# A three-stage kernel (attention, experts, dense layer): a later wait on ScalarE, a turned expert loop, and a dense layer whose two matmul kinds alternate in longer runs

## The chip, the cores and the metric

The kernel runs on one core of a Trainium2 chip. The metric is the device time of one execution in microseconds, as the median of several. Five engines run side by side, each with its own instruction list: TensorE (PE, matrix products), VectorE (DVE), ScalarE (ACT), GpSimd (POOL) and SyncE (SP, which here only starts transfers). They meet through semaphores.

## The reference, cut to what matters

```python
x = attention(q, k, v)                       # pooled attention + a band of |i-j| < 4
x = reshape(x)                               # 2304 tokens x 512
expert = argmax(x @ w_gate); gate = softmax at that expert      # 8 experts
x[rows of e] = gate * (relu(xe @ w1[e]) @ w2[e])                # 512 -> 1024 -> 512
h = x @ w_in                                 # dense layer, 512 -> 2048
g = where(h >= 1, h, where(h <= -1, 0, (h + 1)**2 / 4))
out = g @ w_out                              # 2048 -> 512
```

All inputs and outputs are float32.

## The kernel before, in words

The first 215 us or so are the attention and the routing, which the change does not touch.

**Split products.** From the expert stage on, each operand stands as a high part and a low part, both in a 32-bit format that PE multiplies at a single pass, and one product is three matmuls: high by high, low by high, high by low (`three`, lines 1303 to 1305). ACT makes the high part of each 128x512 weight chunk (line 675), POOL the low part (line 466), and `lo_done` counts the chunks that are ready.

**The expert stage.** Tokens are sorted by expert into slots of 128 rows; there are up to 25 slots, of which 21 (numbers 0 to 20) are in use with these inputs. For a slot s PE runs four steps: `turn_x` (four transposes of the rows), `hidden` (24 matmuls with 512 columns, into two banks), `turn_h` (eight transposes of the hidden values) and `project` (24 matmuls, into one bank). They are pipelined over slots: after a lead-in, PE's order is hidden(s), turn_x(s+1), project(s-1), turn_h(s), and then hidden(s+1). The loop is `Fori(1, 24)` with an `If(s < end)` around its body, where `end` (20 here) is read from a table; so at the end four trips run through with nothing in them. The last slot stands behind the loop. `weights_of(s)` reads two table entries (which expert, which half of the weight memory) into registers; it stands before each `hidden` and each `project`. DVE, SP and ACT have loops of the same kind. SP stores each slot's rows (line 401), waits for the landing, and after its own empty trips it raises `all_stored` (line 417).

**The dense layer.** The tokens are in six groups of three tiles of 128 rows. For a group, f counts 16 blocks of 128 hidden columns. `hidden2(f)` is 12 matmuls with 384 columns into one of two banks (output name tp). Then a chain makes the activation: DVE clamps (line 1078), ACT squares (line 767), DVE combines (line 1082, `act_done`), ACT casts the high part (line 769), POOL subtracts the low part (line 571, `act_lo`). `rows(f)` is 9 matmuls with 512 columns into three banks, one for each tile (output names sc and pt). PE's order is hidden2(f), then rows(f-2); `hidden2(f)` waits for `act_done` of f-2, because it writes that bank anew. At the end of a group stand rows(13), rows(14), rows(15), and then hidden2 of blocks 0, 1 and 2 of the next group. At f = 8 to 11 PE also turns a quarter of the next group's rows (`turn_x2`, three transposes, line 1384), and DVE splits it (`split_x2`). In the first group ACT and POOL still prepare chunks 8 to 15 of `w_out` between their other work. At a group's end ACT copies the three tiles out (`take_group`, line 762) and POOL scatters them to their rows by three indirect transfers (line 566).

**The wait on all_stored.** Buffers of the dense layer lie where the slots' rows lay until they are stored. ACT waits for `all_stored` ahead of the first group's whole work; DVE waits for it ahead of act_f of f = 2.

The orders are written out by hand; nothing reorders them.

Of the kernel before, what the change touches and what calls it, by code (L numbers as in the profile page):

```python
# [52 lines left out]
KD = DM // P  # L53
# [26 lines left out]
def write_program(nc, ctx, q, k, v, w_gate, w1, w2, w_in, w_out, out, x_nat, y_rows):  # L80
# [516 lines left out]
    def _(act):  # L597
# [157 lines left out]


        def take_group(g):
            if not (isinstance(g, int) and g == 0):
                act.wait_ge(rows_stored, 16 * GT * g)
            for n in range(GT):  # L760
                act.wait_ge(o_full, GT * g + n + 1)
                act.copy(rows_out[:, n, :], o_ps[n][:]).then_inc(o_evac, 1)
# [9 lines left out]
            take_group(g)  # L772

        act.sem_inc(o_evac, GT)
        act.wait_ge(all_stored, 1)
        group(0, True)
        with act.Fori(1, GROUPS) as g:
            group(g)
# [3 lines left out]
    def _(dve):  # L782
# [280 lines left out]
        def split_x2(g, par, k):  # L1063
            n = KD * g + k + 1
            turned = (x2T_first[k] if isinstance(g, int) and g == 0 else x2T_ps[k % 2])[:, 0:GT * P]
            dve.wait_ge(x2T_full, n)
            dve.tensor_copy(x2T[par][:, 0, k, :], turned).then_inc(x2T_hi, 1)
            dve.wait_ge(x2T_hi, n)
            dve.tensor_tensor(x2T[par][:, 1, k, :], turned, x2T[par][:, 0, k, :], ALU.subtract).then_inc(x2T_done, 1)

        def group(g, par, last):


            for f in range(KFF):
                n = KFF * g + f + 1
                src = h2_ps[f % 2][:, 0:GT * P]
                dve.wait_ge(h2_full, n)
                dve.tensor_scalar(clamped[f % 2][:], src, -1.0, 1.0, ALU.max, ALU.min).then_inc(clamp_done, 1)  # L1078
                dve.wait_ge(square_done, n)
                if isinstance(g, int) and g == 0 and f == 2:  # L1080
                    dve.wait_ge(all_stored, 1)
                dve.scalar_tensor_tensor(act_f[f % 4][:], src, -1.0, clamped[f % 2][:], ALU.max, ALU.add).then_inc(act_done, 1)  # L1082
                if not last:
                    if 8 <= f < 8 + KD:
                        split_x2(g + 1, 1 - par, f - 8)

        dve.wait_ge(y_stored, 16 * 12)
        for k in range(KD):
# [11 lines left out]
    def _(pe):  # L1100
# [206 lines left out]
        def weights_of(s):  # L1307
            c = pe.value_load(slot_cs[0:1, bass.ds(s, 1)], min_val=0, max_val=E - 1)
            par = pe.value_load(slot_par[0:1, bass.ds(s, 1)], min_val=0, max_val=1)
            return c, par  # L1310
# [4 lines left out]
        def turn_x(s):  # L1315
            pe.wait_ge(xs_done, s + 1)
            if not (isinstance(s, int) and s == 0):
                pe.wait_ge(xT_done, s)
            for k in range(KD):
                e = pe.transpose(xT_ps[:, k * P:(k + 1) * P], xs[:, k * P:(k + 1) * P], ident[:])  # L1320
            e.then_inc(xT_full, 1)

        def hidden(s, c, par):
            pe.wait_ge(xT_done, s + 1)
            if not (isinstance(s, int) and s == 0):
                pe.wait_ge(relu_done, 2 * s)
            for k in range(KD):
                for half in range(2):
                    n = 2 * k + half
                    pe.wait_ge(lo_done, NCH * c + n + 1)  # L1330
                    e = three(h_ps[half][:], lambda part: xT[:, part, k * P:(k + 1) * P],
                              lambda part: chunk(par, part, n), k == 0, k == KD - 1)
                    if k == KD - 1:
                        e.then_inc(h_full, 1)
# [25 lines left out]
        turn_h(0)  # L1360
        keep_clock(sc[1], SPARE // 2)

        def slot(s, last):
            hidden(s, *weights_of(s))
            if not last:
                turn_x(s + 1)
            project(s - 1, *weights_of(s - 1))
            turn_h(s)

        end = pe.value_load(last_slot, min_val=TILES - 1, max_val=SLOTS - 1)  # L1370
        with pe.Fori(1, SLOTS - 1) as s:
            with pe.If(s < end):
                slot(s, False)
        slot(end, True)

        def turn_x2(g, par, k):
            first = isinstance(g, int) and g == 0
# [23 lines left out]
                          lambda part: x2T[par][:, part, k, :], k == 0, k == KD - 1)  # L1401
            e.then_inc(h2_full, 1)

        def rows(g, f):
            pe.wait_ge(act_lo, KFF * g + f + 1)
            if isinstance(g, int) and g == 0:
                pe.wait_ge(lo_done, NCH * (E + 1) + f + 1)
            for i in range(GT):
                if f == 0:
                    pe.wait_ge(o_evac, GT * g + i + 1)  # L1410
                e = three(o_ps[i][:], lambda part: act_s[f % 4][:, part, i * P:(i + 1) * P],
                          lambda part: wts[:, 1, part, f * CH:(f + 1) * CH], f == 0, f == KFF - 1)
                if f == KFF - 1:
                    e.then_inc(o_full, 1)

        def group(g, par, last):
            for f in range(KFF + 2):
                if f < KFF:
                    hidden2(g, par, f)
                if f >= 2:  # L1420
                    rows(g, f - 2)
                if not last and 8 <= f < 8 + KD:
                    turn_x2(g + 1, 1 - par, f - 8)

        group(0, 0, False)
        with pe.Fori(0, GROUPS // 2 - 1) as i:
            group(2 * i + 1, 1, False)
            group(2 * i + 2, 0, False)
        group(GROUPS - 1, 1, True)


_INS = ["q", "k", "v", "moe_w_gate", "moe_w1", "moe_w2", "moe2_w_in", "moe2_w_out"]
# [19 lines left out]
```

## Time and profile before

| | |
|---|---|
| median of 3 runs | 918.72 us (917.51 to 921.9) |
| profiled execution, its own time | 921.8 us |
| its span | 919.9 us |
| mean granted PE clock | 0.982 |
| PE busy | 871.2 us, 95% of the span |
| POOL, DVE, ACT busy | 49%, 49%, 40% |

All times in rows are microseconds from the span's start. PE's matmuls overlap, so the distance between starts tells the pace, and not the duration that a row shows. A bracket at the end of a timeline row is the time in which the engine stood idle ahead of it, and what ended it; "issue" means that the profile shows nothing that it waited for. A bracket may be short of the distance between starts, since the rows' durations include the draining of the last matmul. L-numbers are lines of the kernel.

### The profile page before, as it was taken

To read this page: it belongs to the slowest core of one execution; us is meant where nothing else is said; L and a number is where in the kernel's file an instruction comes from. 1 tells how busy PE (TensorE), PEld (TensorE's weight loads), DVE (VectorE), ACT (ScalarE), POOL (GpSimd) and SP (SyncE) were. 2 spreads that over 40 slices of the span, in tenths; PEclk is the share of its full clock that TensorE was granted. 3 is DMA by queue.
4 is the path that set the end of the run, shared out by engine and by line. 5 is a ranking of instruction groups with operands and counts; after the bars stand their busy time and mean duration, and the time that the engine had idled before them with its cause. 6 is when DMAs were issued, how large, how long until landed. Compare 5 with 4: busy or idle time off the path is not lost.

```text
span 919.9 us, 17885 instructions
## 1 busy us (share of the span) xinstructions
PE 871.2 (95%) x5190; PEld 750.4 (82%) x5191; DVE 447.7 (49%) x1192; ACT 369.2 (40%) x1013; POOL 450.2 (49%) x470
## 2 busy tenths in 40 slices
PE   6999999956998999999998999999999999999995
PEld 5878888845785888888877998999989999899995
DVE  3888888866554545554544242242242242242221
ACT  5888888841322443234222423323223223223222
POOL 4556555665987886588444631421422322322322
PEclk9999999986999999999999999999999999999998
DMA  7355666444776665466434200100200100200000
GB/s 159 78 136 139 148 146 167 116 120 115 217 231 170 197 197 163 128 199 205 137 115 119 101 1 1 70 1 0 70 1 1 69 0 0 69 0 0 35 1 35
DMA packets 109992, 88.71 MB, mean 96 GB/s; under 512 B 67904, under 2 KB 81728, under 8 KB 109952
## 3 DMA queue, kind: packets, MB, share of 16 engines
q10 hardware_dynamic: 23040, 41.95, 15.4%
q1 hardware_dynamic: 83472, 34.87, 14.5%
q0 software_dynamic: 3440, 11.38, 3.9%
q8 instruction: 22, 0.36, 0.2%
q14 instruction: 18, 0.15, 0.0%
HBM read 73.07 MB, written 15.10 MB: 96 GB/s over the span
## 4 chain that ended last, share of the span: by engine, by line
PE 85%; POOL 5%; DMA 3%; issue 3%; DVE 2%; ACT 1%; SPq 0%; ACTq 0%; POOLq 0%; DVEq 0%
PE tp L1303 10%; PE tp L1305 10%; PE tp L1304 10%; PE sc L1138 5%; PE pt L1305 5%; PE pt L1304 5%; PE pt L1303 5%; PE xo L1303 4%; PE xo L1305 3%; PE xo L1304 3%; POOL wts L466 3%; PE tp L1215 3%; PE sc L1304 2%; PE sc L1305 2%; PE sc L1303 2%
## 5 line engine op out<-in xcount | busy, mean ns | idle before, releaser
L571 POOL TENSOR_TENSOR act_s<-act_f,act_s 128x384 fp32r<-128x384 f32 x96 | 97.4, 1015 | 285.5 <-ACT act_s L769 285.4
L466 POOL TENSOR_TENSOR wts<-stage,wts 128x512 fp32r<-128x512 f32 x160 | 205.3, 1306 | 64.7 <-ACT wts L675 58.8
L675 ACT CAST wts<-stage 128x512 fp32r<-128x512 f32 x160 | 98.5, 621 | 206.6 <-DMA stage<-in_moe_w 90.9
L1078 DVE TENSOR_SCALAR clamped<-tp 128x384 f32<-128x384 f32 x96 | 53.5, 558 | 195.9 <-PE tp L1305 195.9
L767 ACT ACTIVATE clamped<-clamped,mhalf 128x384 f32<-128x384 f32 x96 | 59.2, 617 | 217.8 <-DVE clamped L1078 208.4
L1303 PE MATMUL tp<-x2T,wts 128*128 128x384 f32 x384 | 132.1, 344 | 2.7 <-DVE act_f L1082 2.7
L1305 PE MATMUL tp<-x2T,wts 128*128 128x384 f32 x384 | 129.8, 338 | 0.0
L1304 PE MATMUL tp<-x2T,wts 128*128 128x384 f32 x384 | 129.5, 337 | 0.0
L1082 DVE SCALAR_TENSOR_TENSOR act_f<-tp,clamped 128x384 f32<-128x384 f32 x96 | 53.5, 558 | 68.9 <-ACT clamped L767 68.9
L1303 PEld LDWEIGHTS tp<-x2T,wts 128*128 128x128 f32 x384 | 72.6, 189 | 6.5 <-DVE act_f L1082 3.0
L1303 PE MATMUL tp<-wts,xT 128*128 x168 | 68.7, 409 | 7.6 <-POOL wts L466 4.9
L1305 PE MATMUL pt<-wts,act_s 128*128 128x512 f32 x192 | 75.8, 395 | 0.0
L1304 PE MATMUL pt<-wts,act_s 128*128 128x512 f32 x192 | 75.5, 393 | 0.0
L1304 PEld LDWEIGHTS tp<-x2T,wts 128*128 128x128 f32 x384 | 72.7, 189 | 2.8
L1303 PE MATMUL pt<-wts,act_s 128*128 128x512 f32 x192 | 74.5, 388 | 0.0
L616 ACT ACTIVATE prob<-prob,nmax 96x112 f32<-96x112 f32 x192 | 71.8, 379 | 4.0 <-DVE nmax L809 2.9
L769 ACT CAST act_s<-act_f 128x384 fp32r<-128x384 f32 x96 | 49.3, 514 | 59.9 <-DVE act_f L1082 59.9
L1305 PEld LDWEIGHTS tp<-x2T,wts 128*128 128x128 f32 x384 | 72.6, 189 | 0.0
L1303 PE MATMUL xo<-wts,hT 128*128 x168 | 67.5, 402 | 2.1 <-issue 1.6
L1304 PE MATMUL tp<-wts,xT 128*128 x168 | 66.2, 394 | 0.0
L1305 PE MATMUL tp<-wts,xT 128*128 x168 | 66.1, 394 | 0.0
L1305 PE MATMUL xo<-wts,hT 128*128 x168 | 65.7, 391 | 0.0
(187 smaller groups left out, 1678.0 us busy)
## 6 DMA issues: line engine op xcount, KB each, us to landing
stage<-in_moe_w ACTq DMA_DIRECT2D x128, 256.0 KB, 3.0
y_rows<-xg SPq DMA_DIRECT2D x21, 260.0 KB, 3.5
vw<-in_v SPq DMA_DIRECT2D x96, 56.0 KB
x<-y_rows SPq DMA_DIRECT2D x6, 780.0 KB, 4.5
qn<-in_q SPq DMA_DIRECT2D x32, 144.0 KB, 3.3
kn<-in_k SPq DMA_DIRECT2D x32, 144.0 KB, 3.2
v<-in_v SPq DMA_DIRECT2D x16, 288.0 KB
x_nat<-xb SPq DMA_DIRECT2D x16, 288.0 KB, 4.0
```

The source lines that it names most:

```text
L466: pool.tensor_tensor(wts[:, par, 1, cols], stage[:, n % STG, :], wts[:, par, 0, cols], ALU.subtract).then_inc(lo_done, 1)
L571: pool.tensor_tensor(act_s[f % 4][:, 1, :], act_f[f % 4][:], act_s[f % 4][:, 0, :], ALU.subtract).then_inc(act_lo, 1)
L616: e = act.activation(prob[par][g][:, i, :], prob[par][g][:, i, :], ACT.Exp, bias=nmax[par][:, 3 * g + i:3 * g + i + 1], scale=-1.0, accum_ ...
L675: act.copy(wts[:, par, 0, n * CH:(n + 1) * CH], stage[:, n % STG, :]).then_inc(hi_done, 1)
L767: act.activation(clamped[f % 2][:], clamped[f % 2][:], ACT.Square, bias=mhalf[:], scale=0.5).then_inc(square_done, 1)
L769: act.copy(act_s[f % 4][:, 0, :], act_f[f % 4][:]).then_inc(act_hi, 1)
L1078: dve.tensor_scalar(clamped[f % 2][:], src, -1.0, 1.0, ALU.max, ALU.min).then_inc(clamp_done, 1)
L1082: dve.scalar_tensor_tensor(act_f[f % 4][:], src, -1.0, clamped[f % 2][:], ALU.max, ALU.add).then_inc(act_done, 1)
L1138: e = pe.matmul(sc[g % 2][0:TQ, i * W:(i + 1) * W], qT[par][D * hh:D * hh + D, TQ * t:TQ * t + TQ], kT[par][D * hh:D * hh + D, WSTART[t]:W ...
L1303: pe.matmul(o, stationary(0), moving(0), start=start, stop=False)
L1304: pe.matmul(o, stationary(1), moving(0), start=False, stop=False)
L1305: return pe.matmul(o, stationary(0), moving(1), start=False, stop=stop)
```

## The change

ACT's wait for `all_stored` goes from ahead of the first group to that group's `take_group`. In the expert stage hidden(1) is drawn ahead of PE's loop, and a trip is now turn_x(s+1), project(s-1), turn_h(s), hidden(s+1); behind the loop stand project(end-1) and turn_h(end). In the dense layer PE's f goes in steps of two: hidden2(f), hidden2(f+1), rows(f-2), rows(f-1); the turns stand at f = 8, 10, 12, 14, and DVE's splits at f = 9, 11, 13, 15. In the last group the last six triples of matmuls are reordered: block 14 for tiles 0 and 1, block 15 for tile 0, block 14 for tile 2, block 15 for tiles 1 and 2.

```diff
@@ ACT
         def take_group(g):
-            if not (isinstance(g, int) and g == 0):
+            if isinstance(g, int) and g == 0:
+                act.wait_ge(all_stored, 1)
+            else:
                 act.wait_ge(rows_stored, 16 * GT * g)
...
         act.sem_inc(o_evac, GT)
-        act.wait_ge(all_stored, 1)
         group(0, True)
@@ DVE
-                    if 8 <= f < 8 + KD:
-                        split_x2(g + 1, 1 - par, f - 8)
+                    if f >= 9 and f % 2 == 1:
+                        split_x2(g + 1, 1 - par, (f - 9) // 2)
@@ PE
-        def slot(s, last):
-            hidden(s, *weights_of(s))
-            if not last:
-                turn_x(s + 1)
-            project(s - 1, *weights_of(s - 1))
-            turn_h(s)
-
         end = pe.value_load(last_slot, min_val=TILES - 1, max_val=SLOTS - 1)
+        hidden(1, *weights_of(1))
         with pe.Fori(1, SLOTS - 1) as s:
             with pe.If(s < end):
-                slot(s, False)
-        slot(end, True)
+                turn_x(s + 1)
+                project(s - 1, *weights_of(s - 1))
+                turn_h(s)
+                hidden(s + 1, *weights_of(s + 1))
+        project(end - 1, *weights_of(end - 1))
+        turn_h(end)
...
-        def rows(g, f):
+        def rows(g, f, tiles=range(GT)):
...
-            for i in range(GT):
+            for i in tiles:
...
         def group(g, par, last):
-            for f in range(KFF + 2):
+            for f in range(0, KFF + 2, 2):
                 if f < KFF:
                     hidden2(g, par, f)
-                if f >= 2:
+                    hidden2(g, par, f + 1)
+                if f >= 2 and not (last and f >= KFF):
                     rows(g, f - 2)
-                if not last and 8 <= f < 8 + KD:
-                    turn_x2(g + 1, 1 - par, f - 8)
+                    rows(g, f - 1)
+                if not last and 8 <= f < 8 + 2 * KD:
+                    turn_x2(g + 1, 1 - par, (f - 8) // 2)
...
         group(GROUPS - 1, 1, True)
+        rows(GROUPS - 1, KFF - 2, (0, 1))
+        rows(GROUPS - 1, KFF - 1, (0,))
+        rows(GROUPS - 1, KFF - 2, (2,))
+        rows(GROUPS - 1, KFF - 1, (1, 2))
```

## Rows read from the trace of the kernel before

**Rows 1.** PE's waits: releaser, total us, times, longest us.
```profile
PE tp L1303 <- POOL wts L466: 4.9, 9, 1.5
```
**Rows 2.** Timeline at the first dense group: start, duration, engine, what, [idle].
```profile
500.36 0.56 DVE L1078 TENSOR_SCALAR clamped<-tp 128x384 f32<-128x384 f32 x1 [1.29 <-PE tp L1305]
...
501.99 0.34 PE L1305 MATMUL tp<-x2T,wts 128*128 128x384 f32 x1
...
503.75 0.61 ACT L767 ACTIVATE clamped<-clamped,mhalf 128x384 f32<-128x384 f32 x1 [9.36 <-SPq L417]
...
504.40 0.56 DVE L1082 SCALAR_TENSOR_TENSOR act_f<-tp,clamped 128x384 f32<-128x384 f32 x1 [3.48 <-ACT clamped L767]
...
505.01 0.62 PE L1303 MATMUL tp<-x2T,wts 128*128 128x384 f32 x1 [2.68 <-DVE act_f L1082]
...
508.76 0.40 PE L1303 MATMUL sc<-wts,act_s 128*128 128x512 f32 x1
```
**Rows 3.** The windows view: busy time by engine, granted clock, DMA share, GB/s.
```profile
477.00:484.00 7.00, 7.00 (x24) 5.57 (x25) 1.18 (x3) 0.00 (x0) 0.00 (x0) 0.76 0.02 7
505.00:508.30 3.30, 3.29 (x10) 3.29 (x11) 0.97 (x2) 2.56 (x5) 2.72 (x3) 0.52 0.93 301
```
**Rows 4.** The chain of waits: the last slot's store.
```profile
499.35 2.10 DMA y_rows<-xg
```
**Rows 5.** PE's timeline at the loop's end, slots 19 and 20.
```profile
474.08 1.03 PE L1343 MATMUL pt<-ident,hs 128*128 128x128 f32 x8
476.96 0.49 PE L1303 MATMUL tp<-wts,xT 128*128 x1 [1.84 <-issue]
...
484.18 0.39 PE L1303 MATMUL xo<-wts,hT 128*128 x1
...
489.62 1.03 PE L1343 MATMUL pt<-ident,hs 128*128 128x128 f32 x8
```
**Rows 6.** The same in the trip whose hidden step had waited for POOL's weights.
```profile
294.17 0.60 PE L1320 MATMUL sc<-ident,xs 128*128 128x128 f32 x4
295.59 0.49 PE L1303 MATMUL xo<-wts,hT 128*128 x1 [0.83 <-issue]
...
301.17 1.03 PE L1343 MATMUL pt<-ident,hs 128*128 128x128 f32 x8
301.95 0.48 PE L1303 MATMUL tp<-wts,xT 128*128 x1
```
**Rows 7.** PE's timeline at the end of the first group: blocks' first matmuls.
```profile
564.42 0.39 PE L1303 MATMUL sc<-wts,act_s 128*128 128x512 f32 x1
...
566.50 0.39 PE L1303 MATMUL sc<-wts,act_s 128*128 128x512 f32 x1
...
570.58 0.33 PE L1303 MATMUL tp<-x2T,wts 128*128 128x384 f32 x1
...
572.69 0.33 PE L1303 MATMUL tp<-x2T,wts 128*128 128x384 f32 x1
...
574.77 0.41 PE L1303 MATMUL tp<-x2T,wts 128*128 128x384 f32 x1
...
576.95 0.39 PE L1303 MATMUL sc<-wts,act_s 128*128 128x512 f32 x1
```
**Rows 8.** PE's timeline around one turn in the second group.
```profile
604.15 0.49 PE L1384 MATMUL sc<-ident,x 128*128 128x128 f32 x3
604.40 0.42 PE L1303 MATMUL tp<-x2T,wts 128*128 128x384 f32 x1
...
606.57 0.39 PE L1303 MATMUL sc<-wts,act_s 128*128 128x512 f32 x1
```
**Rows 9.** Timelines of ACT and POOL at the kernel's end.
```profile
909.17 0.59 ACT L762 COPY rows_out<-sc 128x512 f32<-128x512 f32 x1 [2.46 <-PE sc L1305]
...
910.59 1.01 POOL L566 DMA_INDIRECT out_rows<-rows_out,tok_i  x1 [2.78 <-ACT rows_out L762]
911.90 0.97 POOL L566 DMA_INDIRECT out_rows<-rows_out,tok_i  x1 [0.30 <-issue]
```

## The prediction

> **What bounds the kernel now.** I read the page first: PE is busy for 95% of the span, and in the dense stage its digits stand at 9 throughout while no other engine passes 50%. So the end is set by PE, and only three things can move it: PE's idle time, its clock, and the pace at which its matmuls follow each other. The waits view then tells how little idle time is left. The largest in the two stages that the change touches is nine waits for POOL's weights, 4.9 us together, the longest 1.5 [rows 1]; the reader should see in the other two (2.68 us for DVE's act_f [rows 2], 1.84 us of issue [rows 5]) that each is a single event, so the timeline around each one tells its cause. Behind both, the windows view shows the granted clock down: mean 0.52 over 505 to 508.3, which is the 1.2 GHz level, and 0.76 over 477 to 484, a mix of the two levels [rows 3].
>
> **Part A, ACT's wait.** The clamp of f = 0 ended at 500.36 + 0.56 = 500.92. ACT squared it only at 503.75, when SP raised all_stored [rows 2]; SP's last store had been issued at 499.35 and landed 2.10 later, at 501.45 [rows 4], and 2.3 us went on its empty trips. DVE's act_f came at 504.40, and PE, whose last matmul before had started at 501.99 and which would have gone on 0.17 later at 502.16, began the third block at 505.01 [rows 2]: 2.85 us lost. Its twelve matmuls then took 508.76 - 505.01 = 3.75 us at the low clock [rows 2, 3], where the same third block of the next group took 576.95 - 574.77 = 2.18 [rows 7]. With the wait moved, the square follows the clamp at once: 500.96, act_f at about 501.6 to 502.2, PE at about 502.25. That is the usual start of a group, where the third block follows with next to no stall (572.69 to 574.77 is a full block, and the first matmul of the third shows some 0.1 of wait) [rows 7]. New end of that block: 502.16 + 2.18 = 504.34, against 508.76: **4.4 us**.
> What is late next: DVE still waits for all_stored ahead of act_f of f = 2. That block's clamp can't start before its 12 matmuls end (about 504.5) and act_f follows some 1.3 later, about 505.8; the flag stands at 503.75. Two microseconds of cover, so this wait costs nothing, and an expert stage that ends earlier moves both alike. Queued behind ACT's moved wait is only the copy of the first group's tiles, 60 us later. Cast and chunk work of f = 0 also comes earlier, and the later chunks' loads with it. Bounds: 0, if the other wait took over; 4.4. I take 4.4.
>
> **Part B, the turned loop.** PE's matmuls are the same ones in the same order; what moves is where the loop's edge, its test, and the empty trips stand. At the usual edge (turn_h, edge, two table reads, hidden) PE loses nothing: eight transposes from 301.17, and hidden at 301.95 [rows 6]. So the sequencer runs ahead of the array by at least the edge and two reads. At the loop's end it has four empty trips as well, and there the transposes from 474.08 end their turn at 8 x 0.109 = 0.87 later, 474.95, and hidden starts at 476.96 [rows 5]: 2.0 us lost. How far ahead it is, in instructions, the trace doesn't show, but it cancels: before, the last instructions ahead of the empty trips are eight transposes at 0.11 us; now they are matmuls of hidden at 0.227 (5.44 us for 24, 484.18 to 489.62 [rows 5]). A lead of between 8 and 24 matmuls is worth 8 x (0.227 - 0.109) = 0.95 us more than before. The stall shrinks from 2.0 to about **1.05 us**. The lead itself: SP's four empty trips took 2.3 [rows 2, 4], two reads take 0.8 to 1.4 (idle between turn_x and project behind a wait, 294.17 to 295.59 [rows 6]), so some 3.4 us, less the stall of 2.0: 1.4 us ahead, that is 8 transposes and 2 or 3 matmuls, inside those limits.
> Then the clock. After 2.0 us of nothing behind 0.87 us of transposes, hidden took 484.18 - 476.96 = 7.22 us, at a mean granted clock of 0.76 [rows 3, 5]; a hidden step at full clock takes about 5.55 (24 x 0.231, the pace of these steps). The pause at 294.17 (transposes, then 0.83 us idle and a start 1.0 late) was followed by a project step of 5.58 us, 295.59 to 301.17 [rows 6], which is the full level. A stall of 1.05 with dense matmuls on both sides is nearer to that one: I take the clock as kept, gaining 1.67. Bounds 0 and 1.67.
> Price: in the trip whose hidden step waits for POOL chunk by chunk, the sequencer is not ahead. Now the edge comes right behind it, ahead of turn_x and project's two reads, and adds itself to the 295.59 start: a trip's edge is about the 2.3/4 = 0.6 us that SP took for an empty one [rows 4]; I take 0.45, bounds 0 and 0.6. Everything ahead of that trip is absorbed by POOL, whose low parts wait for gathers and not for PE [rows 1]. Sum of B: 0.95 + 1.67 - 0.45 = **2.2 us**, bounds -0.6 and 3.6.
>
> **Part C, longer runs.** The distances between blocks' first matmuls show a price for changing kind. rows(13), right behind a hidden2, took 566.50 - 564.42 = 2.08; rows(14) and (15), behind rows, 570.58 - 566.50 = 4.08, 2.04 each. hidden2(0) behind rows took 572.69 - 570.58 = 2.11, hidden2(1) behind hidden2 574.77 - 572.69 = 2.08 [rows 7]. The finer distances fit: behind a change, and there alone, some ten matmuls are irregular. So a change costs 0.041 us into rows and 0.025 into hidden2, to within the 10 ns of a row. Before, a group has 14 of each; now 7 of each. Saved: 7 x 0.066 = 0.46 us a group. Against it, the fourth turn now stands between rows(13) and rows(14). A turn is 0.25, and hidden2 behind it 2.17 (604.15, 604.40, 606.57 [rows 8]); rows behind transposes may cost 5.58 - 5.44 = 0.14 [rows 5, 6] over an undisturbed block, so this turn costs about 0.07 more than it did. Five groups at 0.39 and the last at 0.46: **2.4 us**. Bounds: 0, if the irregularity belongs to something that runs beside; 2.8 above. Waits: hidden2(f+1) writes a bank whose act_f comes 2.0 us after its block's end; in the middle of a group 8 us pass, at its start hidden2(3) follows the stall of hidden2(2) by 2.18, so no more than 0.1 a group. act_lo(f) has more time than before. DVE stands at odd f from 9 on until the turn comes, some 2 us after its act_f; nobody waits for it meanwhile, the split (1.2 us) ends before the next clamp's operand. The next x2 load starts from POOL's f = 4 as before, some 20 us ahead of its turn.
> The Trainium skill (TensorE: Matmul & The Clock Gate, Back-to-back issue gap) gives a warm matmul's spacing as N / 2.4 ns plus about 2.5, a function of the columns alone. By that, order is free and part C is 0; with its figures a pair of blocks would be 12 x 162.5 + 9 x 215.8 = 3.9 us, an estimate from that page, where the trace has 2.11 + 2.08 = 4.19. I go by the trace; the page's case is the second rival.
>
> **Part D, the tail.** ACT copied tile 0 at 909.17; POOL's first scatter started at 910.59, the next 1.31 later at 911.90 [rows 9], and a third at that spacing, while tiles come every 9 matmuls / 3 = 0.68 us. So POOL's row of three is the bound and its start is what counts. Tile 0 is now full three matmuls earlier, 3 x 0.227 = **0.7 us**; tiles 1 and 2 come as before and still find POOL busy (tile 1's scatter can start at 911.2 at the earliest, the new row wants it at 911.2). Bounds 0 and 0.7.
>
> **Sum.** 4.4 + 2.2 + 2.4 + 0.7 = 9.7 us. The profiled execution took 921.8 (span 919.9 and 1.9 around it), which gives 912.1; it is 3.1 above the median of the runs, and the steps that the change touches are not of the kind that varies, so I take 918.7 - 9.7 = **909.0** for the median.
>
> **Rivals.**
> 1. *The stall at the loop's end stays, with its low clock.* The lead is longer than 24 matmuls (then it holds the eight transposes as before) or the clock falls after 1 us all the same. B is then -0.45, the time 909.0 + 2.6 = 911.6. Against it: the lead worked out above. The Trainium skill speaks for it: TensorE: Matmul & The Clock Gate (Architectural detail) gives the engine a queue of 64, and 32 pairs of load and matmul would hold both. By that page the time is this rival's.
> 2. *Changing kind costs nothing by itself*, C is 0: 911.4. For it, that I infer from two blocks in each group where the other engines are also doing other things; against it, that ACT's copies beside rows(15) left its pace alone.
> 3. *Both*: 914.0.
> 4. *The other side: the edge becomes visible in every trip.* In place of POOL-bound trips alone, each trip shows up to 1.0 us of idle, as at 294.17 [rows 6], because the edge, the wait for turn_x's rows and the two reads for project come close together. 19 trips x 1.0 = 19, less the gains: about 918.7 - 9.7 + 19 = 928. It outweighs the gains from 0.5 us a trip on. Against it: before, edge and both reads stood close together behind only eight short transposes, at no cost; now the edge stands behind 24 long ones.
> 5. *More than forecast*: the stall at the end vanishes and the edge costs nothing, 907.5.
>
> **Chances.** Forecast 0.56, rival 1 0.17, rival 2 0.12, both 0.04, rival 4 0.03, rival 5 0.08. Between 905.5 and 913 lies all but the cases "both" and 4, with something for the scatter of runs (917.51 to 921.9 before): that is the range. A median of this kernel tells about 0.5%, 4.6 us, from no change. Faster than 914.1 come all cases but 4 and half of "both": 0.92; within 0.5% 0.05, slower 0.03.
>
> **What would show it.** A: ACT's first square at about 0.1 us behind its clamp, no DVE wait at PE's third block, and no low clock there; wrong if DVE's act_f of f = 2 waits for SP. B: idle of about 1 us between hidden(20) and project(19), both at full clock; and project(4) some 0.45 later behind its gated hidden step. C: pairs of blocks at 4.19 and 4.12 us; wrong if second blocks take 2.11 and 2.08. D: POOL's first scatter 0.7 us earlier against PE's last matmul. The forecast is wrong as a whole if PE shows issue waits in most trips, or if a step's gain turns up as waits for act_lo or x2T.

## The result and the profile after

Over seven runs of each, the changed kernel took 913.42 us in the median (912.28 to 930.98) against 920.47 for the kernel before (917.51 to 936.62). The ratio is 0.9921, with an interval of 0.9902 to 0.9939: 7.3 us less, between 5.6 and 9.0. The forecast was 9.7 us less, 909.0, with a range that ended at 913.0. The time lies 0.4 us outside it. Of the 4.4 us between 909.0 and 913.4, 1.75 are the base (918.72 was the median of three runs, 920.47 that of seven), and 2.65 are gain that did not come, by the medians (2.4 by the ratio).

In the profiled execution of the changed kernel, one of the slow ones of the seven, the attention stage, which the change doesn't touch, took 16 us longer (span 928.5 us), so its rows are read here by the distances between them, never by where they stand.

PE is still the bound. From the page of the changed kernel, each engine's busy time and share:

```profile
PE 883.8 (95%) x5190; PEld 761.3 (82%) x5191; DVE 450.6 (49%) x1192; ACT 369.5 (40%) x1013; POOL 450.0 (48%) x470
```

**The first dense group** (PE's and ACT's and DVE's timelines; start, duration), which answers to [rows 2]:

```profile
515.64 0.34 PE L1304 MATMUL tp<-x2T,wts 128*128 128x384 f32 x1
...
515.92 0.56 DVE L1079 TENSOR_SCALAR clamped<-tp 128x384 f32<-128x384 f32 x1 [1.29 <-PE tp L1306]
...
516.51 0.62 ACT L769 ACTIVATE clamped<-clamped,mhalf 128x384 f32<-128x384 f32 x1 [8.00 <-DVE clamped L1079]
...
517.77 0.44 PE L1304 MATMUL tp<-x2T,wts 128*128 128x384 f32 x1
```

ACT squares 0.03 behind DVE's clamp (515.92 + 0.56 = 516.48), where before it waited 2.8 us for SP's flag. The third block starts 517.77 - 515.64 = 2.13 behind the second, where an unhindered one takes 2.08: the 2.68 us stall has become some 0.05. The window below shows the clock at full level there, where [rows 3] had 0.52.

**The expert loop's end** (PE's timeline), answering to [rows 5]:

```profile
492.29 1.03 PE L1344 MATMUL pt<-ident,hs 128*128 128x128 f32 x8
493.07 0.48 PE L1304 MATMUL tp<-wts,xT 128*128 x1
...
498.39 0.39 PE L1306 MATMUL tp<-wts,xT 128*128 x1
499.64 0.49 PE L1304 MATMUL xo<-wts,hT 128*128 x1 [0.86 <-issue]
...
505.21 1.03 PE L1344 MATMUL pt<-ident,hs 128*128 128x128 f32 x8
```

hidden(20) follows the eight transposes 0.78 later, with no pause. Its last matmul starts at 498.39, the next would follow 0.227 later, and project(19) starts at 499.64: a stall of 1.02 us, forecast 1.05. project(19) then takes 505.21 - 499.64 = 5.57. That is the full clock, but 0.13 more than the 5.44 that it took before [rows 5], when no stall stood ahead of it. The windows view of the same kernel (busy time by engine, granted clock, DMA share, GB/s) shows both places at full clock, and one where it isn't, the trip that waits for weights:

```profile
301.00:304.00 3.00, 3.00 (x8) 1.86 (x8) 1.05 (x2) 1.44 (x3) 3.00 (x3) 0.50 0.52 145
498.00:508.00 10.00, 8.72 (x49) 7.03 (x47) 3.70 (x6) 4.36 (x8) 8.11 (x7) 1.00 0.59 178
517.00:520.00 3.00, 3.00 (x19) 2.67 (x17) 1.68 (x3) 1.75 (x5) 1.66 (x2) 1.00 0.36 87
```

**The weight-bound trip** (PE's timeline after, then hidden(5)'s last matmul before), answering to [rows 6] and [rows 1]:

```profile
310.31 0.40 PE L1306 MATMUL tp<-wts,xT 128*128 x1
310.72 0.65 PE L1321 MATMUL sc<-ident,xs 128*128 128x128 f32 x4
312.58 0.49 PE L1304 MATMUL xo<-wts,hT 128*128 x1 [1.20 <-POOL wts L466]
```

```profile
293.94 0.39 PE L1305 MATMUL tp<-wts,xT 128*128 x1
```

project(4) starts 312.58 - 310.72 = 1.86 behind the group of four turns, where it was 1.42: 0.44 later. The turns themselves start later too, 0.41 behind hidden(5)'s last matmul for 0.23. From that matmul to project it is 2.27 us for 1.65, 0.62 more. The row names POOL, which makes chunk after chunk without a break in this stretch. But project's own chunks, of slot 4's expert, come ahead in POOL's order of those that hidden(5) had just waited for, so they can't be what it waits for. What changed between the two steps is the loop's edge.

In the waits view, project's waits put down to issue are four (1.6 us together, the longest 0.9) where they were three (1.6, the longest 0.8). The three of before were the weight-bound trip and two other trips, 0.41 and 0.33, which no row of the forecast named. Of the four, 0.86 is the loop's end, and the rest (0.43, 0.18 and 0.16) stand in other trips again.

**A usual pair of blocks** (PE's timeline in the second group), answering to [rows 7]:

```profile
590.03 0.39 PE L1304 MATMUL sc<-wts,act_s 128*128 128x512 f32 x1
...
592.11 0.39 PE L1304 MATMUL sc<-wts,act_s 128*128 128x512 f32 x1
...
594.15 0.33 PE L1304 MATMUL tp<-x2T,wts 128*128 128x384 f32 x1
...
596.25 0.34 PE L1304 MATMUL tp<-x2T,wts 128*128 128x384 f32 x1
...
598.33 0.39 PE L1304 MATMUL sc<-wts,act_s 128*128 128x512 f32 x1
```

rows takes 2.08 and then 2.04, hidden2 2.10 and then 2.08. The first of each pair pays the change of kind, the second doesn't.

**The tail** (ACT's, POOL's and PE's timelines; the last two rows are of the kernel before), answering to [rows 9]:

```profile
914.03 1.01 POOL L571 TENSOR_TENSOR act_s<-act_f,act_s 128x384 fp32r<-128x384 f32 x1 [1.06 <-ACT act_s L771]
...
917.77 0.59 ACT L764 COPY rows_out<-sc 128x512 f32<-128x512 f32 x1 [3.82 <-PE sc L1306]
...
919.19 1.01 POOL L566 DMA_INDIRECT out_rows<-rows_out,tok_i  x1 [4.14 <-ACT rows_out L764]
919.39 0.39 PE L1306 MATMUL pt<-wts,act_s 128*128 128x512 f32 x1
...
921.81 0.97 POOL L566 DMA_INDIRECT out_rows<-rows_out,tok_i  x1 [0.30 <-issue]
```

```profile
910.11 0.39 PE L1305 MATMUL pt<-wts,act_s 128*128 128x512 f32 x1
...
913.17 0.97 POOL L566 DMA_INDIRECT out_rows<-rows_out,tok_i  x1 [0.30 <-issue]
```

The first scatter now starts 0.20 ahead of PE's last matmul (919.19 against 919.39); before it started 0.48 behind it (910.59 [rows 9] against 910.11). The last one starts 2.42 behind it instead of 3.07 (rounding apart, 913.17 - 910.11). So 0.65 to 0.68 came, of the 0.68 forecast.

### The profile page after: what moved, and what is told of

It reads as the page before. It is cut to its first block, busy times and chain, and to the rows that moved or that the text cites. A ratio compares the mean times of both kernels' runs of the same rounds, so it can differ in the third digit from the quotient of the medians.

```text
span 928.5 us, 17866 instructions
## 1 busy us (share of the span) xinstructions
PE 883.8 (95%) x5190; PEld 761.3 (82%) x5191; DVE 450.6 (49%) x1192; ACT 369.5 (40%) x1013; POOL 450.0 (48%) x470
## 4 chain that ended last, share of the span: by engine, by line
PE 81%; POOL 10%; issue 4%; DMA 2%; DVE 2%; ACT 0%; SPq 0%; POOLq 0%; ACTq 0%; DVEq 0%
PE tp L1304 9%; PE tp L1306 9%; PE tp L1305 9%; POOL wts L466 7%; PE sc L1139 6%; PE pt L1306 5%; PE pt L1305 5%; PE pt L1304 5%; PE tp L1216 3%; PE xo L1304 3%; PE tp L1124 3%; PE xo L1306 3%; PE xo L1305 3%; PE xo L1203 2%; PE sc L1148 2%
## 5 line engine op out<-in xcount | busy, mean ns | idle before, releaser
L1304 PE MATMUL xo<-wts,hT 128*128 x168 | 67.8, 403 | 3.8 <-issue 1.6
L482 POOL TENSOR_TENSOR prob<-prob,rden 96x336 f32<-96x336 f32 x64 | 46.3, 744 | 44.2 <-DVE rden L831 44.2
```

The lines of the kernel that those rows point to most:

```text
L1304: pe.matmul(o, stationary(0), moving(0), start=start, stop=False)
```

## The experiments

Eleven kernels ran, each beside executions of the kernel before. In "us less" the ratio and its interval are turned into microseconds with the median of those executions (920.07 to 920.95).

| kernel | what it is | us | ratio (interval) | us less |
|---|---|---|---|---|
| e1_wait | before + ACT's wait moved | 915.57 | 0.9952 (0.9937 to 0.9966) | 4.4 |
| e2_loop | before + turned loop | 917.53 | 0.9995 (0.9977 to 1.0013) | 0.5 |
| e3_pairs | before + longer runs | 918.93 | 0.9987 (0.9977 to 0.9998) | 1.2 |
| e8_tail | before + last matmuls reordered | 920.35 | 0.9999 (0.9990 to 1.0008) | 0.1 |
| e4_after_again | the changed kernel | 912.47 | 0.9918 (0.9904 to 0.9933) | 7.5 |
| e6_after_old_loop | changed, with the old loop | 913.31 | 0.9921 (0.9906 to 0.9937) | 7.3 |
| e5_after_early_copy | changed, DVE copies early | 909.77 | 0.9883 (0.9865 to 0.9901) | 10.8 |
| e7_before_early_copy | before, DVE copies early | 917.64 | 0.9969 (0.9958 to 0.9981) | 2.9 |
| e9_recut_early_copy | third cut of the loop, copies early | 909.61 | 0.9886 (0.9871 to 0.9901) | 10.5 |
| e10_recut | third cut alone | 912.94 | 0.9920 (0.9906 to 0.9933) | 7.4 |
| e11_old_loop_early_copy | changed, old loop, copies early | 911.27 | 0.9907 (0.9891 to 0.9922) | 8.6 |

### Part A alone: e1_wait

```diff
 def take_group(g):
-    if not (isinstance(g, int) and g == 0):
+    if isinstance(g, int) and g == 0:
+        act.wait_ge(all_stored, 1)
+    else:
...
 act.sem_inc(o_evac, GT)
-act.wait_ge(all_stored, 1)
 group(0, True)
```

> The kernel before with only ACT's wait moved into take_group. Theory 1 (the prediction's part A): 4.4 us less than before, PE's third block of the first dense group follows with at most 0.1 us of stall and at full clock. Rival (another wait takes its place, DVE's own wait for all_stored): 0 to 1 us less, and DVE's act_f of f = 2 is the instruction that waits for SP.

Measured: 4.4 us less (3.1 to 5.8). The first dense group, from its first matmul to that of the next, went from 72.61 to 68.29 us, 4.32 less; a usual group takes 68.21 here. In this profile no act_f of DVE waits for SP (91 wait for ACT's square, five for nothing that the profile shows), so DVE's own wait costs nothing. The theory of part A holds. This run also showed something else, at the loop's end, where the PE loop is still the old one (PE's timeline, then the windows view):

```profile
492.87 0.49 PE L1304 MATMUL tp<-wts,xT 128*128 x1 [1.88 <-issue]
...
498.46 0.39 PE L1304 MATMUL xo<-wts,hT 128*128 x1
```

```profile
490.00:496.00 6.00, 4.12 (x23) 3.33 (x22) 3.33 (x5) 0.00 (x0) 0.00 (x0) 1.00 0.13 47
```

The stall is the one of [rows 5], 1.88 for 1.84, yet hidden(20) takes 498.46 - 492.87 = 5.59 us for 7.22, and the clock stays at full level. The loss of 1.6 us that the forecast wanted back isn't there in every execution.

### Part B alone and taken back: e2_loop, e6_after_old_loop

In outline:

```diff
-for s in 1..: if s < end: hidden(s); turn_x(s+1); project(s-1); turn_h(s)
-slot(end, True)
+hidden(1)
+for s in 1..: if s < end: turn_x(s+1); project(s-1); turn_h(s); hidden(s+1)
+project(end-1); turn_h(end)
```

> The kernel before with only PE's expert loop turned. Theory 1 (the prediction's part B): 2.2 us less. Theory 2 (formed from the trace after): the end of the loop gains 2.6 us as forecast, but the trips lose most of it, 0.43 at the trip behind the weight wait and another 0.6 to 1.2 spread over trips in which DVE's copy of the slot's rows comes late, because project starts 2.0 us behind such a copy where it started 1.9 behind it; net 0 to 1.5 us less, and each pause between turn_x and project in the trace stands at 2.0 us behind the copy's end. Rival (chance of one execution: the gathers landed later in the profiled run): the late copies are the same in number and the pauses as before.

> The changed kernel with PE's expert loop as before. The prediction's part B (the turned loop is worth 2.2 us): 7.5 us less than before, 2.2 more than the changed kernel. Theory B (the turned loop gains 1.1 us at its end, pays 0.43 at the weight-bound trip and some 0.9 in longer pauses, and what else it gains, 1.65 us, comes only in executions whose clock fell after the long stall): 6.5 to 7.2 less than before, within 1 us of the changed kernel, and the stall ahead of hidden(20) is 1.84 us whether the clock falls or not.

Measured: e2 0.5 us less (from 1.2 more to 2.1 less), and e6, which takes the turn back, has the same ratio as the changed kernel. That speaks against 2.2, but not sharply. e2's times stand in two bunches, seven of 916.6 to 917.8 with a mean granted clock of 0.984 or more, and five of 920.4 to 925.7 with 0.983 or less; so its median is 2.5 us under that of before, while the ratio says 0.5. What part B is worth has to come from the rows. e2's profile also shows the start of the dense layer, where ACT's wait stands as before (PE's timeline and the windows view):

```profile
501.36 0.44 PE L1303 MATMUL tp<-x2T,wts 128*128 128x384 f32 x1 [2.67 <-DVE act_f L1082]
...
503.57 0.39 PE L1303 MATMUL sc<-wts,act_s 128*128 128x512 f32 x1
```

```profile
501.00:505.00 4.00, 3.65 (x19) 3.38 (x20) 1.88 (x4) 3.04 (x6) 3.08 (x3) 1.00 0.92 283
```

The same stall of 2.67 us, and the block behind it takes 503.57 - 501.36 = 2.21, not 3.75: the clock wasn't lost behind this one either. Its first group is 71.08 us long, not 72.61.

### Part C alone and part D alone: e3_pairs, e8_tail

```diff
-for f in range(KFF + 2):
+for f in range(0, KFF + 2, 2):
     hidden2(g, par, f)
+    hidden2(g, par, f + 1)
     rows(g, f - 2)
+    rows(g, f - 1)
```

The turns and DVE's splits stand in e3 where they stand in the changed kernel.

> The kernel before with only the dense layer's longer runs and DVE's moved splits. Theory 1 (part C, a change of kind costs 0.041 into rows and 0.025 into hidden2): 2.4 us less, a usual group takes 67.8 to 67.9 us from first to first matmul where it took 68.2. Rival (changing kind costs nothing): same time, groups at 68.2.

Measured: 1.2 us less (0.2 to 2.1). By its profile a usual group goes from 68.20 to 67.89 us, the first from 72.61 to 72.29, the last from 66.73 to 66.27 (last start to last start). That is 0.32 + 4 x 0.31 + 0.46 = 2.0, at the upper end of the interval.

```diff
-if f >= 2:
+if f >= 2 and not (last and f >= KFF):
     rows(g, f - 2)
...
 group(GROUPS - 1, 1, True)
+rows(GROUPS - 1, KFF - 2, (0, 1)); rows(GROUPS - 1, KFF - 1, (0,))
+rows(GROUPS - 1, KFF - 2, (2,)); rows(GROUPS - 1, KFF - 1, (1, 2))
```

> The kernel before with only the last six triples of matmuls reordered. Part D (POOL's row of three scatters starts 0.68 us earlier against PE's last matmul): 0.7 us less than before, of 918.7 a ratio of 0.9993. Rival (the end is set by the last tile's copy and scatter): first scatter earlier, third at the same place, no change.

Measured: nothing that can be told, 0.1 us less (from 0.7 more to 0.9 less). The rows of e8's last matmuls tell why (POOL's and PE's timelines):

```profile
905.72 1.01 POOL L571 TENSOR_TENSOR act_s<-act_f,act_s 128x384 fp32r<-128x384 f32 x1 [3.18 <-ACT act_s L769]
906.32 0.39 PE L1305 MATMUL pt<-wts,act_s 128*128 128x512 f32 x1
906.79 0.50 PE L1303 MATMUL sc<-wts,act_s 128*128 128x512 f32 x1
```

PE reaches rows(15) for tile 0 three matmuls earlier than it did, but POOL makes its low part only at 905.72 + 1.01 = 906.73, and PE starts at 906.79 where it could have at 906.55 (906.32 and a pace of 0.227). The last group grows from 66.73 to 67.09 us, 0.36. The scatters did move: the first starts 0.21 ahead of PE's last matmul and the last 2.42 behind it, 0.65 better than before, as in the changed kernel. So by the rows some 0.3 us are left of the 0.65, inside the interval; neither the 0.7 expected nor the rival, whose last scatter stays in place, is what happened. In the changed kernel hidden2(14) and (15) both stand ahead of rows(12), so that the same low part is ready by 915.04 (914.03 + 1.01), 1.8 us ahead of its use, and the last group shows no such growth (66.27, as in e3). Part D gives its 0.65 in full only on top of part C.

### The changed kernel again: e4_after_again

> The changed kernel once more, unchanged, for a second profile and more runs. Theory 1 (the forecast sum): 9.7 us less than before. Theory 2 (trips lose most of what the loop's end gains): 7.5 to 9 us less. Step from the first expert step to the first dense step (PE's hidden(0) to hidden2(0)): 271.6 to 272.5 by theory 1, 273.2 to 274.5 by theory 2, where it took 274.2 before.

Measured: 7.5 us less (6.2 to 8.8), the lower end of theory 2. The groups are 68.04, four of 67.87 to 67.93, and 66.27 us long: those of the profile after to 0.03. From hidden(0) to hidden2(0) it is 272.6 us, between what the two theories asked for (272.5 at most, 273.2 at least), so this step decides nothing: one execution with or without a low clock differs by more. The profile was read for the pauses that no part explains. Wherever a project step starts late, outside the weight-bound trip, DVE's copy of the next rows (line 1012) had ended late and project follows its end by 2.0 us; rows of such a trip stand in the next section.

### DVE's copy taken out of the way: e5_after_early_copy, e7_before_early_copy

```diff
 def slot(s, last):
-    if not last: copy_rows(s + 1)
     relu(s)
     if not last:
         split_x(s + 1)
+        with dve.If(s + 1 < end):
+            copy_rows(s + 2)
     take_y(s - 1); split_h(s)
...
+copy_rows(2)   # ahead of the loop
```

> The changed kernel, and DVE copies the rows of slot s+2 right behind split_x(s+1), before take_y(s-1) and split_h(s), and not at the head of the next trip. Theory A (project follows no earlier than 2.0 us behind the end of DVE's copy, and the copy is late where it runs beside POOL's weight work): all pauses between turn_x and project behind the weight-bound trip fall to 0.03 us, 1.5 to 2.1 us less than the changed kernel, 9 to 9.5 less than before. Rival (the pauses are PE's table reads and have nothing to do with the copy): pauses stay, same time as the changed kernel.

> The kernel before, with DVE's earlier copy as in the run above and nothing else. Theory A: the pauses behind the weight-bound trip, 1.0 to 1.2 us in sum with the old loop, go; 1 us less than before, up to 1.7 where a slot ahead of the weight-bound trip had one too, as POOL's weights absorb those. Rival (pauses are table reads): same time as before.

Measured: e5 10.8 us less than before (9.1 to 12.4), some 3.2 less than the changed kernel in ratio; e7 2.9 less (1.7 to 3.9). Both are more than expected (1.5 to 2.1 under the changed kernel; 1 to 1.7 under before). The rows bear out the smaller figure: from the last matmul of hidden(5) to turn_h(20) it is 192.5 us in e5 against 194.4 in e4, 1.9 less. Where the other 1.3 of e5's timings come from isn't known; e5 was timed in four executions only. In e5 a copy beside POOL (whose line 466 runs from 404.86 to 411.33 here) is still long (DVE's and PE's timelines), but nobody waits for it:

```profile
406.32 1.38 DVE L1012 COPY xs<-xg 128x512 f32 x1
...
416.46 0.60 PE L1322 MATMUL sc<-ident,xs 128*128 128x128 f32 x4
416.81 0.48 PE L1305 MATMUL xo<-wts,hT 128*128 x1
```

project follows the four turns 0.35 behind their start, with no pause, in every trip after the weight-bound one. The pauses that the copy removes there sum to 1.2 in the profile of before. The rest of e7's 2.9 may be the clock, which in its profile stays full at the loop's end; that one profile doesn't show it for all its executions.

### A third cut of the loop, and the old one, with and without early copies: e9, e10, e11

A trip here is turn_h(s), hidden(s + 1), turn_x(s + 2), project(s), so that the edge stands between project and turn_h, away from the wait for DVE's rows. In outline, without the shifted counts of one semaphore (relu_done):

```diff
+hidden(1); turn_x(2); project(0)
 for s in 1..: if s + 1 < end:
-    turn_x(s+1); project(s-1); turn_h(s); hidden(s+1)
+    turn_h(s); hidden(s+1); turn_x(s+2); project(s)
+turn_h(end-1); hidden(end)
 project(end-1); turn_h(end)
```

e9_recut_early_copy is this with the early copy, e10_recut without it; e11_old_loop_early_copy is the changed kernel with the old loop and the early copy.

> The changed kernel with DVE's earlier copy, and PE's expert loop cut at a third place: a trip is turn_h(s), hidden(s+1), turn_x(s+2), project(s), so the edge and the empty trips stand behind project's 24 matmuls and no table read follows them at once. Theory C (where the edge stands next to the reads, both are paid behind a wait): against the run with the early copy and the turned loop, the pause at the weight-bound trip falls from 1.51 back to 1.1 and the 1.0 us stall ahead of project(19) goes, 1.2 to 1.5 us less, about 12 less than before. Rival (the stall follows the empty trips wherever they stand): it stands ahead of turn_h(19) at 1 us, gain 0.4 or nothing.

> The same third cut without DVE's earlier copy. Theory C: project starts 1.9 us behind a late copy as with the first loop, not 2.0, so the pauses are about 0.1 each shorter than in the changed kernel; 1.4 to 2 us less than the changed kernel. Rival (the 0.1 belongs to the later code, not to the edge): 2.0 as in the changed kernel.

> The changed kernel with the expert loop as before and DVE's earlier copy. With the pauses out of the way what the turned loop is worth shows by itself: 1.14 at its end, less 0.43 at the weight-bound trip, and 1.65 more in those executions whose clock fell behind the 1.84 us stall. Expected 0.7 to 2.4 more than the run with the early copy and the turned loop, so 8 to 10 less than before; hidden(20) takes 5.6 us or 7.2 us, nothing between.

Measured: e9 10.5 us less (9.1 to 11.9), the same as e5, where about 12 was expected; e10 7.4 less (6.2 to 8.6), the same as the changed kernel, where 1.4 to 2 under it was expected; e11 8.6 less (7.2 to 10.0), some 2.2 short of e5, as expected (0.7 to 2.4), with hidden(20) at 5.6 us. PE's timeline of e9, the weight-bound trip and the loop's end:

```profile
300.07 0.60 PE L1323 MATMUL sc<-ident,xs 128*128 128x128 f32 x4
301.51 0.49 PE L1306 MATMUL xo<-wts,hT 128*128 x1 [0.84 <-issue]
...
478.82 1.03 PE L1346 MATMUL pt<-ident,hs 128*128 128x128 f32 x8
480.41 0.49 PE L1306 MATMUL tp<-wts,xT 128*128 x1 [0.56 <-issue]
```

The weight-bound trip's pause is back at 1.44 as in [rows 6], and a part of what was gained at the loop's end went: hidden(20) starts 1.59 behind the eight transposes, not 0.78. e10 shows the other half (DVE's and PE's timelines):

```profile
465.77 1.55 DVE L1012 COPY xs<-xg 128x512 f32 x1
...
469.24 0.49 PE L1305 MATMUL xo<-wts,hT 128*128 x1 [0.34 <-issue]
...
475.36 1.09 PE L1345 MATMUL pt<-ident,hs 128*128 128x128 f32 x8 [0.38 <-issue]
477.55 0.49 PE L1305 MATMUL tp<-wts,xT 128*128 x1 [1.10 <-issue]
```

A late copy (end 467.32) is followed by project 1.92 later, as with the old loop (1.87 to 1.92), and not 2.01 as with the turned one. But the third cut pays elsewhere in e10: the project step that had waited for the late copy is the one ahead of the empty trips, and PE pauses twice behind it, 0.38 and 1.10. From project(18) to turn_h(20) e10 needs 19.3 us, against 18.5 with the turned loop and 18.2 in e9. That takes back the 0.6 that the weight-bound trip gains.

## Why the prediction was right in three parts and wrong in one

| part | forecast | timed alone | by the rows |
|---|---|---|---|
| A, ACT's wait | 4.4 | 4.4 (3.1 to 5.8) | 4.3, of it 1.5 clock; 4.0 in the mean |
| B, turned loop | 2.2 | 0.5 (-1.2 to 2.1) | about 0.6 |
| C, longer runs | 2.4 | 1.2 (0.2 to 2.1) | 2.0 |
| D, the tail | 0.7 | 0.1 (-0.7 to 0.9) | 0.65, in full only with C |

By the rows the four parts are 4.0 + 0.6 + 2.0 + 0.65 = 7.3 us, where 7.3 and 7.5 were measured. Of the 2.4 that are missing, 1.6 are part B's. On the base that the forecast used, 918.7, a gain of 7.3 would have given 911.4, inside the range and next to the 911.4 and 911.6 of rivals 2 and 1. That would have been luck: neither rival's mechanism is what happened, and the gain was a quarter short all the same.

**Part A was right**, its mechanism and its size, and the wait that remains on DVE cost nothing. What the prediction took as certain, and isn't, is the clock's share. The stall ahead of the third block, 3.0 us from start to start, was followed by the low clock in four of the five profiles that have it (before, e3, e7, e8) and not in e2. So over many executions the part is worth nearer 4.3 - 1.5 / 5 = 4.0.

**Part C was right in mechanism and 0.4 too large.** The second blocks run at 2.08 and 2.04 as forecast, and rival 2, which gave the pattern no price, is out. A usual group gained 0.31, though, not 0.39. The turn between rows(13) and rows(14) cost what the prediction allowed for it. In the fourth turn of the changed kernel (PE's timeline):

```profile
577.13 0.49 PE L1383 MATMUL xo<-ident,x 128*128 128x128 f32 x3
577.38 0.48 PE L1304 MATMUL sc<-wts,act_s 128*128 128x512 f32 x1
...
579.53 0.39 PE L1304 MATMUL sc<-wts,act_s 128*128 128x512 f32 x1
...
581.57 0.33 PE L1304 MATMUL tp<-x2T,wts 128*128 128x384 f32 x1
```

rows(14) behind the transposes takes 2.15, 0.11 over an undisturbed block's 2.04 (0.14 was allowed). The missing 0.08 lies in two small terms that the sum left out. hidden2(3), which now follows the late hidden2(2) at once, takes 2.11 in the usual groups of e4 in place of 2.08; the prediction gave this "no more than 0.1 a group" and entered nothing. And the three hidden2 that still follow a turn take 2.17 to 2.20 there, where they took 2.17 before.

**Part D was right, 0.65 for 0.68**, with a condition that the prediction didn't name: the low parts must be ahead, which part C sees to.

**Part B failed**, in three terms of its sum; the fourth held, 1.0 for 0.95.

The first is "I take the clock as kept, gaining 1.67". What it says of the changed kernel held: the stall was 1.02 us for 1.05, and the clock was kept, in all four profiles with the turned loop (after, e2, e4, e5). The error is on the side of before. From project(18) to the first transpose of turn_h(20), PE needs 18.49 to 18.52 us in those four. With the old loop it needs 21.06 to 21.13 in four profiles (before, e3, e6, e8) and 19.48 to 19.52 in three (e1, e7, e11), where the same stall of 1.84 to 1.89 us was not followed by a fallen clock. So 1.0 us is gained always, and 1.6 more only where an execution would have lost it: 4 of 7, 0.9 in the mean. [Rows 3] showed one execution, and its 1.67 was entered in full, with the words that "the steps that the change touches are not of the kind that varies". They are: the two fallen clocks of that execution cost 1.6 and 1.5 us, and it stood 3.1 above the median. The timings agree that the clock varies from one execution to the next: of the executions of before beside e1 to e4, the five with a mean granted clock of 0.980 took 921.0 us in the mean, the five with 0.984 918.5.

The second is the price in the weight-bound trip, put at 0.45 and in fact 0.6, the bound that the prediction gave. From the last matmul of hidden(5) to project(4) it is 1.64 to 1.67 us in the nine profiles with the edge elsewhere and 2.25 to 2.27 in the four with it there, and hidden(6) starts 0.6 later as well.

The third is a price at nothing. The sum charged the edge in one trip only, but it costs 0.1 us in each trip whose copied rows come late. With the old loop or the third cut, project starts 1.87 to 1.93 behind the end of such a copy, with the turned loop 1.98 to 2.03. And the sum of the pauses behind late copies in the rest of the stage was 0.97 to 1.88 (mean 1.30) in the five profiles with the old loop and late copies, and 1.69 to 2.38 (mean 1.97) in the three with the turned one: 0.67 more. Of this, 0.1 a trip in four to six trips is shown, some 0.5. The rest may be chance, since these profiles are few and the counts vary from three to six, and e10 had 2.30 with the edge elsewhere.

Put together, B is 1.0 + 0.9 - 0.6 - 0.67 = 0.6. The whole stretch says the same: from the last matmul of hidden(5) to turn_h(20), the three profiles with the turned loop and late copies take 194.5 us in the mean, the five with the old loop 195.5, or 195.1 with the clock's loss at 4 of 7 in place of their 4 of 5. The changed kernel also showed a low clock behind the wait for weights, in the window 301:304 above; PE waits for POOL there, and from hidden(0) to the end of hidden(5) it took 70.7 us where the other profiles have 69.8 to 70.5.

This is rival 4 in small. It asked for an edge that shows in every trip once it stands next to the wait for turn_x's rows and the two reads of project; the trips where it shows are only those where PE has no lead. Rival 1 is out: a stall that shrinks from 1.84 to 0.86 of issue is what a lead of 8 to 24 matmuls gives. The Trainium skill's page TensorE: Matmul & The Clock Gate (Architectural detail) gives the engine a queue of 64 instructions, which would have kept the stall; the traces here speak against that much lead in this loop.

Two slips in the working changed nothing. The 5.44 us read off [rows 5] as hidden's are project(19)'s. And the chances named for "faster than 914.1" add up to 0.95, not 0.92.

**What makes the rows late** was not in the prediction at all, though it costs before as well. POOL's, DVE's and PE's timelines of the profile after:

```profile
356.20 3.82 POOL L466 TENSOR_TENSOR wts<-stage,wts 128x512 fp32r<-128x512 f32 x3
...
358.16 0.69 DVE L1031 TENSOR_TENSOR hT<-pt,hT 128x512 fp32r<-128x512 f32 x1
358.83 1.48 DVE L1012 COPY xs<-xg 128x512 f32 x1
...
361.36 0.60 PE L1321 MATMUL sc<-ident,xs 128*128 128x128 f32 x4
362.28 0.49 PE L1304 MATMUL xo<-wts,hT 128*128 x1 [0.33 <-POOL wts L466]
```

The copy needs 1.48 us while POOL makes weights. e5 takes the copy out of the way and no such pause is left; so that the copy makes those pauses is shown. That the edge, where it is adjacent, costs 0.1 is shown too, by e10, which moves it away with the late copies kept. How it comes about is an account that fits the rows and that no run tests alone: PE's sequencer stands at the wait for the copied rows and loses its lead, the four turns and then project's two table reads are issued with nothing ahead of them, and what the reads take is a pause of the array. Why an adjacent edge costs 0.1 us behind a short wait and 0.6 behind a long one stays open.

**The better version.** e5, the changed kernel with the copy one step earlier, beats both: 0.9883 of before (0.9865 to 0.9901), against 0.9918 and 0.9921 for the changed kernel. Against the old loop with early copies (e11: 0.9907, 0.9891 to 0.9922) it is 2.2 us ahead, but the intervals overlap, and the rows of the two profiles, both at full clock, give 0.35 (192.51 against 192.86 from hidden(5) to turn_h(20)), close to the 1.0 - 0.6 of the sum above. So turning the loop pays a little once nothing makes PE wait for rows, and more in executions that would lose the clock. The third cut should have given 1.2 to 1.5 us more on top; e9's profile shows 0.9 less than e5's over the same stretch, the timings nothing.

## What to carry to other kernels

A loss at a low clock that one profile shows behind a stall of a few microseconds may be absent from the next execution: enter it in a forecast by the share of profiles that have it, and look at more than one before the sum is made. A profiled execution that stands above the median by as much as its own clock losses is a warning of this. When a loop is cut at another place, its edge is paid wherever the sequencer has no lead, so list every trip in which the engine waited for anything short, and not only the largest wait of the page. A reordering at a kernel's end can depend on another part of the change for its operands, so test it on its own and within the whole.

## What the runs showed of the hardware that was not expected

- **A DVE copy beside POOL.** The copy xs<-xg, 128 x 512 floats from SBUF to SBUF, takes 0.42 to 0.43 us when no instruction of POOL's line 466 overlaps it (85 of 91 copies in the thirteen profiles; 0.66 at most). When one is running at the copy's start, the copy ends 0.28 to 0.30 us behind the end of that instruction, in 170 of 174 cases, whether it takes 0.43 us by that or 1.59. In the rows above, 358.83 + 1.48 is 0.29 behind 356.20 + 3.82. DVE's operations that read PSUM keep their 0.68 to 0.69 us beside the same POOL instruction, as at 358.16. The Trainium skill's page SBUF — State Buffer (Terms) says that these two engines share a port pair under an exclusive lock which the loser waits for during a whole instruction; the trace agrees, with the copy's end tied to that of POOL's instruction.
- **The clock after a pause of PE.** The same stall of 1.84 to 1.89 us was followed by the 1.2 GHz level in four of seven profiles, that of 2.67 to 2.69 us in four of five, and the one of 0.86 in none of four. What decides within one kind is left open here.
- **The price of changing kind**: a block of nine 512-column matmuls takes 2.08 behind 384-column ones and 2.04 behind its own kind, one of twelve 384-column ones 2.10 to 2.11 and 2.08. It is there in every group of the profiles before, after, e3 and e4.
